# Expert loop in groups of three pairs, one-hot products inside the last tile's branch, last block by groups of rows

## What is computed

```python
for t in range(S):                     # linear attention, one step per t
    cur = np.einsum('bhd,bhe->bhde', u[None] * kt, vt)
    y[:, :, t] = np.einsum('bhd,bhde->bhe', rt, state + cur)
    state = w[None, :, :, None] * state + np.einsum('bhd,bhe->bhde', kt, vt)
...
do_compute = x @ w_skip > 0            # mixture of 8 experts, for some of the tokens
e_idx = np.argmax(x[do_compute] @ w_gate, axis=1)
h = np.maximum(xc[mask] @ w1[e], 0.0)
out[do_compute] = xc + gate_w * (h @ w2[e])
...
h = x @ w_in                           # dense layer
(h * np.clip(h + 3.0, 0.0, 6.0) / 6.0) @ w_out
```

## Time and profile before

| what | value |
|---|---|
| median of three runs (729.45 to 732.04) | 731.68 us |
| the profiled execution's own time | 736.82 us |
| its span, first to last instruction | 735.0 us |
| mean granted TensorE clock | 0.984 of full speed |
| PE busy, share of the span | 698.5 us, 95% |
| DVE, ACT, POOL busy | 384.8, 324.3, 139.4 us |

### The profile page before, as it was taken

The page is one execution under the profiler, slowest core; times in us unless marked ns, Lnnn a source line. Parts: engine busy times, 40 slices in busy tenths (PEclk is TensorE's granted clock), DMA queues, the critical chain, the costliest instruction groups (busy, mean ns, idle before and its releaser), DMA issues.

```text
span 735.0 us, 13595 instructions
## 1 busy us (share of the span) xinstructions
PE 698.5 (95%) x5103; PEld 638.1 (87%) x5103; DVE 384.8 (52%) x767; ACT 324.3 (44%) x703; POOL 139.4 (19%) x189
## 2 busy tenths in 40 slices
PE   5999999957999999989999999999999999999997
PEld 3888887847999999978999899899899899898896
DVE  5576677565788888656544333433333333333332
ACT  3766667624565555634343232333233233223232
POOL 8647756442222222100000000000000000000000
PEclk9999999977999999999999999999999999999999
DMA  9788788113966666710002000200200020001001
GB/s 155 148 184 166 165 171 171 45 33 118 348 232 209 215 222 216 264 60 1 1 1 86 1 1 1 86 1 1 71 16 1 1 86 1 1 1 43 1 1 43
DMA packets 106986, 65.57 MB, mean 89 GB/s; under 512 B 79938, under 2 KB 102756, under 8 KB 106928
## 3 DMA queue, kind: packets, MB, share of 16 engines
q1 hardware_dynamic: 102864, 60.18, 30.7%
q0 software_dynamic: 2816, 4.60, 2.0%
q10 hardware_dynamic: 1248, 0.02, 0.1%
HBM read 53.69 MB, written 12.80 MB: 90 GB/s over the span
## 4 chain that ended last, share of the span: by engine, by line
PE 90%; ACT 4%; issue 2%; DVE 2%; DMA 1%; POOL 0%; POOLq 0%; DVEq 0%; ACTq 0%; SPq 0%
PE bank_A L876 8%; PE bank_A L877 8%; PE bank_A L875 8%; PE bank_A L813 4%; PE bank_L L875 4%; PE bank_L L877 4%; PE bank_L L876 4%; PE bank_P L875 4%; PE bank_P L876 4%; PE bank_P L877 4%; PE bank_kT L876 3%; PE bank_kT L877 3%; PE bank_kT L875 3%; PE bank_YT L877 3%; PE bank_YT L876 3%; PE bank_YT L875 3%
## 5 line engine op out<-in xcount | busy, mean ns | idle before, releaser
L1264 DVE TENSOR_TENSOR g_lo<-g,g_hi 128x512 fp32r<-128x512 f32 x96 | 66.5, 692 | 67.1 <-ACT g_hi L701 67.1
L701 ACT ACTIVATE g_hi<-g 128x512 fp32r<-128x512 f32 x96 | 60.7, 632 | 73.1 <-DVE g L1262 73.1
L1262 DVE SCALAR_TENSOR_TENSOR g<-cut,bank_A 128x512 f32<-128x512 f32 x60 | 41.2, 687 | 92.8 <-ACT cut L698 92.8
L698 ACT ACTIVATE cut<-bank_A 128x512 f32<-128x512 f32 x60 | 35.8, 597 | 101.4 <-PE bank_A L877 100.8
L877 PE MATMUL bank_A<-mT_hi,wi_lo 128*128 128x512 f32 x180 | 71.0, 394 | 0.0
L876 PE MATMUL bank_A<-mT_lo,wi_hi 128*128 128x512 f32 x180 | 70.9, 394 | 0.0
L875 PE MATMUL bank_A<-mT_hi,wi_hi 128*128 128x512 f32 x180 | 70.0, 389 | 0.0
L590 ACT ACTIVATE bank_A<-ident,own 128x128 f32<-128x128 f32 x192 | 59.2, 359 | 6.1 <-DVE A_sb L1048 3.0
L1262 DVE SCALAR_TENSOR_TENSOR g<-cut,bank_kT 128x512 f32<-128x512 f32 x36 | 24.7, 687 | 66.6 <-ACT cut L698 66.6
L698 ACT ACTIVATE cut<-bank_kT 128x512 f32<-128x512 f32 x36 | 21.5, 597 | 69.7 <-PE bank_kT L877 69.7
L875 PE MATMUL bank_A<-xgT_hi,w_hi 128*128 128x256 f32 x144 | 41.6, 289 | 1.3 <-DVE xgT_lo L1221 1.3
(11 more groups left out here) (240 smaller groups left out, 1852.2 us busy)
## 6 DMA issues: line engine op xcount, KB each, us to landing
raw<-in_moe_w_dram SPq DMA_DIRECT2D x24, 512.0 KB
raw<-in_moe_w_dram SPq DMA_DIRECT2D x7, 1536.0 KB
r_in<-in_r_dram SPq DMA_DIRECT2D x24, 192.0 KB, 4.4
k_in<-in_k_dram SPq DMA_DIRECT2D x24, 192.0 KB, 4.7
v_in<-in_v_dram SPq DMA_DIRECT2D x24, 192.0 KB, 3.5
x_scratch<-y_sb SPq DMA_DIRECT2D x24, 192.0 KB, 2.5
out_dram<-o_sb SPq DMA_DIRECT2D x12, 384.0 KB, 2.8
m_in<-x_scratch SPq DMA_DIRECT2D x5, 768.0 KB, 5.3
```

The costliest lines, as they stand in the source:

```text
L698: eng.activation(cut[f % 2][:, :], p_H[f % 3][:, :], ACT.Relu, bias=0.5, scale=1.0 / 6.0).then_inc(s_cut, 1)
L701: eng.activation(g_hi[f % 4][:, :], g[f % 2][:, :], ACT.Copy).then_inc(s_ghi, 1)
L1262: eng.scalar_tensor_tensor(g[f % 2][:, :], cut[f % 2][:, :], 1.0, p_H[f % 3][:, :], ALU.min, ALU.mult).then_inc(s_g, 1)
L1264: eng.tensor_tensor(g_lo[f % 4][:, :], g[f % 2][:, :], g_hi[f % 4][:, :].bitcast(F32), ALU.subtract).then_inc(s_glo, 1)
```

## The change

`expert_loop` now serves PE too: pair 0 written out, then up to three groups of three pairs, each group under a test of `n_tiles`. With 8 tiles one group runs and two are passed over. In the last tile's branch on each engine: PE makes the one-hot products, half t = 0 for the three banks, then half t = 1; ACT splits 8 pieces of `w_in` and makes `gain_hi` for t = 0 as soon as that half's `yg` is written, and after the loop the pieces 8 to 11 and `gain_hi` for t = 1; DVE makes the four low parts of `w_in` ahead of `yg`, and `gain_lo` of each half directly after its `yg`. In the last block PE finishes steps 14 and 15 for one group of 128 rows after the other, in the order 0, 2, 1, 3; each group is copied and stored (192 KB) by itself.

```diff
+PAIRS = E // 2 - 1
+ROUNDS = -(-(MAXT // 2 - 1) // PAIRS)
+LAST_ROWS = (0, 2, 1, 3)
+HI_EARLY, HI_FIRST, LO_EARLY, LO_FIRST = 8, 12, 4, 6
...
-        def expert_loop(eng, n_tiles, step):
-            for i in range(2):
-                step(i, 0, i)
-            with eng.Fori(1, E // 2) as m:
...
+        def expert_loop(eng, n_tiles, pair):
+            pair(0, 0)
+            with eng.Fori(0, ROUNDS) as group:
+                with eng.If(n_tiles > group * (2 * PAIRS) + 2):
+                    with eng.Fori(group * PAIRS + 1, group * PAIRS + PAIRS + 1) as m:
+                        pair(m * 2, m)
...
 # SP, last block
+                if last:
+                    for t in LAST_ROWS:
+                        half = t // (BT // 2)
+                        eng.wait_ge((s_oA, s_oV)[half], blk + 2 + t % (BT // 2))
+                        eng.dma_start(out[blk * BLK + t * P:blk * BLK + (t + 1) * P, :], o_sb[:, t, :]).then_inc(s_out[half], 16)
+                    return
...
 # ACT, experts
+                with eng.If(n_tiles < j + 2):
+                    eng.wait_ge(s_wi, 16 * W_PARTS)
+                    for f in range(HI_EARLY):
+                        win_hi(f)
+                    eng.wait_ge(s_y2ev, TH * j + 1)
+                    last_gain(0)
...
-            eng.wait_ge(s_wi, 16 * W_PARTS)
-            for f in range(HI_FIRST):
+            for f in range(HI_EARLY, HI_FIRST):
                 win_hi(f)
-            for t in range(TH):
-                eng.wait_ge(s_y2ev, n_tiles * TH)
-                eng.activation(gain_hi[t][:, :], ...
+            eng.wait_ge(s_y2ev, n_tiles * TH)
+            last_gain(TH - 1)
...
 # PE, experts
                 with eng.If(n_tiles < j + 2):
                     first_rows_T()
+                    for t in range(TH):
+                        for kc in range(KC):
+                            a = last_gain(t, kc)
+                            if t == TH - 1:
+                                a.then_inc(s_mT, 1)
...
 # PE, last block
+                if last:
+                    for t in LAST_ROWS:
+                        for f in (G2 - 2, G2 - 1):
+                            eng.wait_ge(s_glo, G2 * blk + f + 1)
+                            a = product(t, f)
+                        a.then_inc(s_O, 1)
+                    return
...
 # DVE, experts
+                with eng.If(n_tiles < j + 2):
+                    for f in range(LO_EARLY):
+                        win_lo(f)
                 wait(eng, s_sc[i], 16 * TH * m)
                 for t in range(TH):
...
+                    with eng.If(n_tiles < j + 2):
+                        last_gain(t)
```

More of the change, by code:

```diff
@@ L45 @@
 W_PARTS = 8
-HI_FIRST, LO_EARLY, LO_FIRST = 12, 4, 6
+HI_EARLY, HI_FIRST, LO_EARLY, LO_FIRST = 8, 12, 4, 6
 SETS = 3
@@ L372, in experts, with load_w_out, pair @@
+            def load_w_out():
+                for part in range(W_PARTS):
+                    own_g = slice(part * G2 // W_PARTS, (part + 1) * G2 // W_PARTS)
+                    eng.dma_start(wo_raw[:, own_g, :], wo_dram[:, own_g, :]).then_inc(s_wo, 16)
+            def pair(j, m):
+                if isinstance(j, int):
+                    with eng.If(n_tiles > 1):
+                        fetch_weights(1, 1)
+                    load_w_out()
                     return
                 with eng.If(n_tiles > j):
-                    e = eng.value_load(plan[0:1, bass.ds(j, 1)], min_val=0, max_val=E - 1)
@@ L375, in experts @@
[L375 to L388, removed]
+                    fetch_weights(j, 0)
+                    with eng.If(n_tiles > j + 1):
+                        fetch_weights(j + 1, 1)
+            expert_loop(eng, n_tiles, pair)
@@ L416, in _ @@
             for done in s_out:
-                eng.wait_ge(done, 16 * (NBLK + 1))
+                eng.wait_ge(done, 16 * (NBLK + BT // 2))
         @block.gpsimd
@@ L894, in first_rows_T, with last_gain @@
                                    is_transpose=True, skip_group_check=True)
+            def last_gain(t, kc):
+                for gain, done in ((gain_hi, s_gain_hi), (gain_lo, s_gain_lo)):
+                    eng.wait_ge(done, t + 1)
+                    a = eng.matmul(p_first_mT[kc], gain[t][:, kc * P:(kc + 1) * P], goes_to[t][:, :], start=False,
+                                   stop=gain is gain_lo and t == TH - 1, skip_group_check=True)
+                return a
             def experts(j, m, i):
@@ L940, in rows_mT, with product @@
                 a.then_inc(s_mT, 1)
+            def product(t, f):
+                tok = slice(t * P, (t + 1) * P)
+                return three(p_O[t][:, 0:D], g_hi[f % 4][:, tok], g_lo[f % 4][:, tok], wo_hi[:, f, :], wo_lo[:, f, :],
+                             f == 0, f == G2 - 1)
             def second(blk, f, first=False):
@@ L982, in _ @@
             eng.sem_inc(s_O, SHIFT)
-            for kc in range(KC):
-                for t in range(TH):
-                    for gain, done in ((gain_hi, s_gain_hi), (gain_lo, s_gain_lo)):
-                        eng.wait_ge(done, t + 1)
-                        a = eng.matmul(p_first_mT[kc], gain[t][:, kc * P:(kc + 1) * P], goes_to[t][:, :], start=False,
-                                       stop=gain is gain_lo and t == TH - 1, skip_group_check=True)
-                a.then_inc(s_mT, 1)
             dense_loop(eng, blocks)
@@ new lines, in experts @@
+                with eng.If(n_tiles > j + 1):
+                    incoming(j + 1, m + i, 1 - i)
+                eng.tensor_copy(last_w[:, :], who[i][:, :, 1].bitcast(F32))
+                eng.tensor_copy(last_id[:, :], who[i][:, :, 0]).then_inc(s_lastid, 1)
+                eng.wait_ge(s_lastid, j + 1)
+                for t in range(TH):
+                    eng.tensor_scalar(goes_to[t][:, :], token[:, :], last_id[:, t:t + 1], None, ALU.is_equal)
+                with eng.If(n_tiles < j + 2):
+                    for f in range(LO_EARLY):
+                        win_lo(f)
@@ new lines, in experts @@
+                wait(eng, s_sc[i], 16 * TH * m)
+                for t in range(TH):
+                    if t < TH - 1:
+                        eng.wait_ge(s_y2t, (TH - 1) * j + t + 1)
+                    else:
+                        eng.wait_ge(s_y2, j + 1)
+                    eng.scalar_tensor_tensor(yg[i][t][:, :], p_y[t][:, 0:D], who[i][:, t, 1:2].bitcast(F32), xg[i][:, t, :],
+                                             ALU.mult, ALU.add).then_inc(s_y2ev, 1)
+                    with eng.If(n_tiles < j + 2):
+                        last_gain(t)
@@ L1278, in _ @@
             eng.sem_inc(s_g, SHIFT)
-            for t in range(TH):
-                eng.wait_ge(s_gain_hi, t + 1)
-                eng.scalar_tensor_tensor(gain_lo[t][:, :], p_y[t][:, 0:D], last_w[:, t:t + 1], gain_hi[t][:, :].bitcast(F32),
-                                         ALU.mult, ALU.subtract).then_inc(s_gain_lo, 1)
-            for f in range(LO_EARLY):
-                win_lo(f)
             for kc in range(KC):
```

145 lines of the change are left out of this document (77 added, 68 removed).

## The result

The change takes 724.59 us (median of five runs, 724.30 to 725.56). The kernel before, in five runs of its own, takes 729.82 (729.04 to 732.04). The ratio is 0.9923, with a 95% interval of 0.9903 to 0.9944: **5.2 us less**, 0.8%, and clear of no change. Of the 3.1 us between forecast and result 1.9 are in the starting point (731.68 was the median of three runs, 729.82 is that of five), and 1.2 in the gain, 5.2 for 4.0.

A forecast was written before the change was run, and what follows sets the result against it. PE was taken to bound the expert tiles, leaving only the seams: 3.3 us before the dense layer plus 0.7 at the end, 4.0 us (bounds 1.9 and 5.4) off the median 731.68, so 727.7 us, range 726.3 to 730.3.

The forecast's parts named there:

- The chain's 1.90 us of issue: Between last tile and dense layer: the chain of waits waited for nothing the profile names, 1.90 us; PE passes over six rounds.
- the loop's end: PE, before the dense layer: 27 control instructions become 14, 2.61 us becomes about 1.35; dense layer starts at 319.2 us.
- The clock's share: One-hot products before the dense layer: full clock, eight products each 0.2 us shorter, about 1.6 of the 3.3 us gain.
- rival B: Seam before the dense layer: clock stays low or was not always low; gain only 2.3 us, 729.4; chance 0.16.
- rival C: Seam before the dense layer: the loop's end is not shorter; gain 2.6 us, 729.1; chance 0.16.
- rival E: Expert tiles lose to added tests what the seams win (2 us on DVE): no change, 729.7 to 731.7; chance 0.07.
- the lower bound: Dense layer's earliest start, 318.73 us, if the loop's end is all hidden while products run; 319.2 was taken.
- The stall on `g_lo`: Last block, PE: three matmuls instead of twelve cover the wait for `g_lo`; PE stalls 0.3 us, 0.4 with the restart.
- the last store's earlier issue: Kernel's end: one store issued at 731.16 us, where the second store was issued at about 731.52; 0.36 us less.
- the last store's way from issue to the end: Kernel's end: a 192 KB store takes 2.5 us in the median, one of 384 KB 2.8; 0.3 us less.
- The low parts' move: DVE, last tile: four low parts, 1.96 us, ahead of `yg`; first `yg` slips some 0.2 us, hidden.
- Rival D: PE passing over two groups: code is fetched at up to five long jumps; at most 4 us slower, 735.7; chance 0.06.

The follow-up runs named there:

- experiment 1: Kernel before with PE's own loop alone in groups of three pairs, one-hot products still behind the loop: 727.49 us, ratio 0.9959 to before.
- experiment 2: Changed kernel with PE's old loop (three rounds taken, six passed over), products in the last tile's branch: 729.09 us, ratio 0.9981 to before.
- experiment 6: Changed kernel with the last block's rows stored in two halves of 384 KB, as before: 731.98 us, ratio 0.9936 to before.
- experiment 4: Changed kernel with DVE's four low parts of `w_in` back behind the loop: 726.96 us, ratio 0.9956 to before.
- experiment 5: Changed kernel with the low parts behind the loop and DVE's loop in its old form, without groups: 732.88 us, ratio 0.9951 to before.
- experiment 7: Changed kernel with old-form loops on all engines and the waits on `mT_lo` and `g_lo` taken out: 733.97 us, ratio 0.9961 to before.
- experiment 10: Changed kernel with PE's loop alone in the old form, jumping over a second copy of its body: 734.32 us, ratio 0.9957 to before.
- experiment 11: Changed kernel with PE's loop alone in the old form, without the second copy and its test: 732.13 us, ratio 0.9917 to before.

## Why the prediction was wrong

**The mechanism was right in the main.** The chain's 1.90 us of issue was the loop's end, the slow products were the clock's, and both are gone. The clock's share was put at about 1.6 us and measured 1.56. The work moved into the branch is hidden on DVE, ACT and PE as argued; rivals B, C and E did not come.

**The loop's end was mis-sized, and counted from the wrong place.** "The 27 took 2.61 us ..., so 14 take about 1.35 us", and the dense layer was to start 1.35 us behind the last product's start. It started 0.97 behind it, 0.11 us from the lower bound (3.51 us from the last transpose; measured 3.62), and what it waited for was the split of the first sum. 2.61 us were what stuck out behind the matmuls already queued; the full price is 0.18 us an instruction (experiments 1 and 2), counted from the last wait ahead. In the change that is the second half's `gain_lo`, done at 308.75, and the loop's end runs from 308.8 to 310.7 us, 1.9 us beside the products. So the step that failed is the one from the lower bound, 318.73, to 319.2: the loop's end does not hold the dense layer at all. Two errors of opposite sign, a price too low and a start too late, nearly cancelled: seam 3.3 forecast, 3.65 measured, and that it came so near is in part luck.

**The end was mis-sized: 0.7 forecast, 1.51 measured.** The stall on `g_lo` and the copies came out as forecast (0.07 us less forecast, 0.01 measured). So, nearly, did the last store's earlier issue: 0.36 us forecast, 0.27 measured (0.01 in the copy, 0.26 behind it). The term that failed is the 0.3 us for the last store's way from issue to the end: it fell by 1.24 us (3.55 to 2.31). Half the size is 0.6 of that (experiment 6), and the other 0.64 came with the spacing of the last two stores, for which the sum had no term: before, they were issued 0.42 us apart (731.07, 731.49), in experiment 6, with stores of the same size, 1.11 us apart. The 0.3 came from the `x_scratch` stores of the earlier trace rows, which go out in the attention stage's traffic; a 192 KB store at the quiet end lands in 1.9 us, as the upper bound's nearest row, 1.6, had suggested.

**The low parts' move was priced at nothing, by its cost alone.** DVE's loop's end was not priced at all, while SP's and ACT's were. With the low parts left in their old place the seam is 1.43 us longer (experiments 4 and 5). The slip of 0.2 us forecast for the first `yg` did not come. The forecast did not suffer, because the change has both edits.

**The range** took its top from rivals B and C and its foot from the sum's larger bounds. The measured gain, 5.2 us, lies within these bounds (5.4); the time does not, because all was counted from a median of three runs, 1.9 us above that of five.

**Rival D** was right in what such a jump costs and wrong that this change makes one that does. The groups' jumps pass over two tiles' code and back without a packet of instructions, 0.2 us each; on PE a jump over a second copy takes 4.1 to 4.2 us, 2.14 us net (experiments 7, 10 and 11). The argument against the rival misread one figure: the twelve jumps of before took 4.6 us, not 2.61, since they began ahead of the last transpose. The rule of the Trainium skill (Runtime: NRT & Kernel Launch, Instruction fetch mechanics), that a taken branch to code outside the fetched pages stalls for a fetch, agrees with experiment 10: one packet of 0.02 MB in 3.13 us. No run here tells why the same jump costs nothing on the other engines (0.07 us at most, experiment 7).

**Left open:** why the clock fell in some of these gaps and not in others (below), and the 0.16 us of the expert tiles, which is less than they vary from run to run.

## What to carry to other kernels

Price a loop's end by counting its control instructions (0.18 us each on PE here) from the last semaphore wait ahead of it, or, where nothing waits, from where they begin in the trace, and subtract the queued work that runs beside it; never scale the idle time that sticks out. On PE, replace rounds that are passed over by groups that reuse the same code, not by a second copy that is jumped over; on DVE the second copy was the shorter end (experiments 4 and 5). Look for such an end on every engine that has work due behind the loop. At a kernel's end the last store counts by itself: make it small and let it go out alone.

## What the runs showed that was not expected

- The clock behind a gap of PE: before, PE idled 2.34 us behind the transposes and the clock fell to 0.50 half a microsecond into the products. In experiment 2 it idled 2.85 us behind products, in experiment 10 2.74 us, and the clock stayed at 1.00 over the next 4 us of each profile; in experiment 7 it fell after 2.52 us. The length of the gap alone does not decide it, and these runs don't show what does.
- One jump over a second copy of a loop's body took 4.2 us on PE, more than twice the end of the groups' loop with its fourteen control instructions, 1.9 us, all of it beside other work; on the other engines such a jump took 0.07 us at most.
